# Two activation buffers declared ahead of the weight buffers, in an attention and MLP kernel

## What is computed

```python
q_bucket, k_bucket = (sum over 6 bits of (x @ proj > 0) * 2**bit for x in (q, k))
scores = where(q_bucket == k_bucket, q @ k.T / 8, -1e9)     # batch 2, 8 heads, 768 x 768, head_dim 64
attn = exp(scores - max); attn = attn / (sum(attn) + 1e-9)
x = (attn @ v), heads side by side                          # 1536 tokens x 512
r = maximum(x @ w_in, 0)                                    # 512 -> 2048
y = (s * r * r + b) @ w_out                                 # 2048 -> 512
out = ((y @ w1) * (y @ w2)) @ w3 @ w_out2                   # 512 -> 1024 -> 1024 -> 512
```

## Time and profile before

| | us |
|---|---|
| median of 3 executions | 785.99 |
| lowest, highest | 784.29, 786.78 |
| profiled execution, its own time | 785.99 |
| its span in the profile | 784.2 |

### The profile page before, as it was taken

One profiled execution on the slowest core, in us unless ns is written; L12 is line 12 of the kernel. 1 busy time (PEld: TensorE's weight loads), 2 busy tenths in 40 slices (PEclk: granted clock), 3 DMA queues, 4 the chain that ended last, 5 costly groups with the idle time before them and its releaser, 6 DMA issues.

```text
span 784.2 us, 11231 instructions
## 1 busy us (share of the span) xinstructions
PE 756.1 (96%) x3680; PEld 625.5 (80%) x3680; DVE 459.7 (59%) x809; ACT 369.3 (47%) x686; POOL 238.9 (30%) x150
## 2 busy tenths in 40 slices
PE   3999999999989899999999999999999999999998
PEld 2788888887778778888888888888887888888886
DVE  4899999999979821277565675666675201210220
ACT  2889998898879933353232232322342211211211
POOL 3347665575566663662021020210112000000000
PEclk9999999999989999999999999999999999999999
DMA  5353334333532223233010110101010000001001
GB/s 148 80 119 82 87 91 113 78 83 85 120 114 61 67 91 107 81 109 106 1 53 1 54 54 0 53 1 53 1 53 1 1 35 20 1 14 40 0 0 54
DMA packets 17680, 45.37 MB, mean 58 GB/s; under 512 B 4946, under 2 KB 6994, under 8 KB 17650
## 3 DMA queue, kind: packets, MB, share of 16 engines
q1 hardware_dynamic: 17650, 44.99, 20.7%
HBM read 37.75 MB, written 3.19 MB: 52 GB/s over the span
## 4 chain that ended last, share of the span: by engine, by line
PE 81%; DVE 7%; ACT 4%; issue 4%; DMA 2%; SPq 1%; POOL 0%; DVEq 0%; ACTq 0%
PE psum L986 54%; PE psum L1073 8%; PE psum L940 6%; PE psum L927 5%; PE psum L916 3%; DVE top L745 3%; PE psum L910 3%; ACT prob L524 2%; DVE pt_lo L759 1%; ACT pt_hi L540 1%; DVE x_lo L863 1%; PE psum L901 1%; DMA stage<-in_w_out 1%; DMA raw<-in_qk 1%; DVE qm L738 1%
## 5 line engine op out<-in xcount | busy, mean ns | idle before, releaser
L759 DVE TENSOR_TENSOR pt_lo<-psum,pt_hi 128x384 fp32r<-128x384 f32 x192 | 97.8, 549 | 12.7 <-ACT pt_hi L540 11.2
L524 ACT ACTIVATE prob<-psum,exp_at 128x768 f32<-128x768 f32 x96 | 96.3, 1003 | 11.2 <-DVE exp_at L752 11.1
L540 ACT ACTIVATE pt_hi<-psum 128x384 fp32r<-128x384 f32 x192 | 84.3, 494 | 20.3 <-PE psum L927 18.9
L745 DVE TENSOR_REDUCE top<-psum 128x1 f32<-128x768 f32 x96 | 90.9, 947 | 4.2 <-PE psum L916 4.0
L632 ACT ACTIVATE relu<-psum 128x512 f32<-128x512 f32 x48 | 28.6, 598 | 131.4 <-PE psum L986 131.4
L986 PE MATMUL psum<-x_hi,w_c 128*128 128x512 f32 (+1 forms) x288 | 88.7, 389 | 0.0
L986 PE MATMUL psum<-x_hi,w_b 128*128 128x512 f32 (+1 forms) x288 | 88.7, 389 | 0.0
L927 PE MATMUL psum<-ident,prob 128*128 128x128 f32 x576 | 83.8, 280 | 4.2 <-DVE pt_lo L759 3.9
L886 DVE TENSOR_TENSOR ab<-psum,a_sb 128x512 f32<-128x512 f32 x24 | 16.6, 691 | 117.8 <-ACT a_sb L682 117.8
L840 DVE SCALAR_TENSOR_TENSOR relu<-psum,relu 128x512 f32<-128x512 f32 x48 | 33.1, 689 | 84.8 <-ACT relu L632 79.8
L403 POOL TENSOR_TENSOR w_b<-stage,w_b 128x1024 fp32r<-128x1024 f32 x18 | 43.7, 2427 | 122.9 <-ACT w_b L551 122.2
(11 more groups left out here) (91 smaller groups left out, 1460.0 us busy)
## 6 DMA issues: line engine op xcount, KB each, us to landing
raw<-in_qk SPq DMA_DIRECT2D x30, 384.0 KB, 5.2
stage<-in_w_out SPq DMA_DIRECT2D x12, 512.0 KB, 3.3
stage<-in_w3t SPq DMA_DIRECT2D x8, 512.0 KB, 3.9
stage<-in_w_in SPq DMA_DIRECT2D x8, 512.0 KB, 3.2
stage<-in_w SPq DMA_DIRECT2D x8, 512.0 KB, 3.3
raw_v<-in_v SPq DMA_DIRECT2D x16, 192.0 KB, 2.7
qm<-both_hi SPq DMA_DIRECT2D x16, 192.0 KB, 2.7
r_sb<-r_rows SPq DMA_DIRECT2D x16, 192.0 KB, 5.4
```

The source lines that it names most:

```text
L524: act.activation(prob[:, t % 3], score[t % 2], ACT.Exp, bias=exp_at[:, t % 2, 1:2], scale=exp_at[:, t % 2, 0:1], accum_out=rsum[:, (t // 6 ...
L540: act.activation(pt_hi[:, u % 2, 3 * part:3 * part + 3, (t % 3) * P:(t % 3 + 1) * P], turned[part].rearrange("p (j q) -> p j q", j=3), ACT ...
L745: dve.tensor_reduce(top[:, t % 2, 1:2], score[t % 2], AX.X, ALU.max, negate=True).then_inc(top_done, 1)
L759: dve.tensor_tensor(pt_lo[at], turned[part].rearrange("p (j q) -> p j q", j=3), pt_hi[at].bitcast(F32), ALU.subtract).then_inc(pt_lo_done, 1)
```

## The change

Two declarations move from behind w_b to the head of the list. x_hi then begins at byte 16,512, x_lo at 41,088, stage at 65,664, ident at 73,856, sb_col at 74,368, w_a at 74,400 and w_b at 107,168. Before, stage began at 16,512, ident at 24,704, sb_col at 25,216, w_a at 25,248, w_b at 58,016, x_hi at 74,400 and x_lo at 98,976. The next buffer begins at 123,552 in both.

```diff
+        x_hi = sb("x_hi", [P, KT, TOK], FR)
+        x_lo = sb("x_lo", [P, KT, TOK], FR)
         stage = sb("stage", [P, 2, WCH], F32)
         ident = sb("ident", [P, P], F32)
         sb_col = sb("sb_col", [P, 2], F32)
         w_a = sb("w_a", [P, 8 * WCH], FR)
         w_b = sb("w_b", [P, 4 * WCH], FR)
-        x_hi = sb("x_hi", [P, KT, TOK], FR)
-        x_lo = sb("x_lo", [P, KT, TOK], FR)
```

## The result

| | before | after |
|---|---|---|
| median of 6 executions, us | 785.13 | 792.94 |
| lowest to highest, us | 783.85 to 786.78 | 791.89 to 794.51 |
| profiled execution, us | 785.99 | 792.57 |
| its span, us | 784.2 | 790.8 |

The kernel is slower by 0.98%: ratio 1.0098, 95% interval 1.0083 to 1.0113, 7.8 us. The forecast was no change.

What follows compares the result with a forecast made beforehand. PE was taken to bound the kernel from 279.5 us on, at 226.7 ns per matmul. All six terms were 0, so 785.99 + 0 = 786.0 us, range 782.6 to 789.0, no change at 0.82.

Steps and rivals of the forecast that it cites:

- What bounds the kernel: PE sets the end from 279.52 us on; 2208 matmuls at 226.7 ns make 500.6 of 504.7 us, hand-over the rest.
- The alignment step: Buffer starts: only x_hi and x_lo change alignment, from 32 past a multiple of 64 onto one; five others keep theirs.
- Term 1: 1152 matmuls streaming x_hi or x_lo, hidden steps and second part: 0, between 15.4 us gained and 16.1 us lost.
- Terms 2 to 6: Weight loads, x_hi/x_lo writes at the hand-over, ACT copies, transfers into stage, register arithmetic for x addresses: each 0.
- The rule weighed: Skill's 215.7 ns per 512-column matmul against 226.7: if start address cost it, 12.7 us gain; 16-byte lines said no change.
- rival A: 64-byte start makes streamed x reads cheaper: in whole 770.6 us, chance 0.03; in part 780.9 us, chance 0.03.
- Rival B: Hidden steps: x directly below busy stage makes 576 matmuls 14 ns longer each, 8.1 us lost, 794.1 us; chance 0.05.
- The sign I had named: MLP matmuls: forecast wrong if paces streaming x and g differ by 2 ns or more; 1152 x 2 ns is 2.3 us.

Runs made afterwards that it cites:

- Experiments 1, 2 and 4: 1: 32-byte pads around x_hi/x_lo, either layout, 792.92 and 793.89 us; 2: one front pad 786.77, shifted x views 791.54; 4: changed kernel, sb_col ahead of x_hi, 784.82.
- experiment 7: Also spelled stream_alone: separate kernel with only matmuls on constant data; total time meaningless; float32r, 512 columns: 226.7 ns at distance 0, 233.4 at 32 and 128.
- low_32: Changed kernel with 32-byte pads ahead of x_hi and behind x_lo, so x begins 32 bytes further up: 792.92 us, ratio 1.0097 to the kernel before.

## Why the prediction was wrong

- **What bounds the kernel** held. PE sets the end from 278 us on, and 1152 of the 2208 matmuls carry the change. One reading in it was loose: the hand-over is 11.3 us of the chain (584.27 to 595.61), not the 4.1 that 504.7 - 500.6 leaves, as 48 of the x matmuls run beside it.
- **The alignment step** failed first. I worked out that 57,888 bytes leave a remainder of 32 modulo 64 and that the weights move by a multiple of 256, and took the streamed operand's own alignment for what could matter. The two moved by different remainders modulo 256 (-32 and 0), and that relation is what costs. Experiments 1, 2 and 4 show it: all operands on a multiple of 64 is fast, the same x address is fast or slow by its weights. (Stage is also not the only one of the five that a transfer fills, sb_col is another; nothing hung on that.)
- **Term 1** is the step that failed in the sum. Its value of 0 came from rows with four streamed buffers and three weight buffers, all at 389 ns. They looked like many placements and were one: every one began at 160 modulo 512. What was constant in them was the very thing that the change altered. The term was 6.7 ns x 1152 = 7.7 us; the upper bound of 16.1 us, borrowed from ACT copies, held it, but I let the range end at 789.0.
- **Terms 2 to 6** held. Weight loads read 188 ns, the hand-over, the ACT copies and the hole at 218 us were the same, and the register-addressed blocks lose 6.7 ns per matmul beside 6.3 (0.91 us over 144) in the one with fixed addresses.
- **The rule weighed.** The Trainium skill's 215.7 ns (TensorE: Matmul & The Clock Gate, section "Wait — 56ns, not 53.3ns?") agrees with this chip for bfloat16: 215.8 ns in experiment 7. For float32r no distance tried gave a pace under 226.7, so those 11 ns were not to be had by moving buffers; rival A was as wrong as the forecast. The 16-byte lines that the Trainium skill states (SBUF — State Buffer, section "Door 1: The DMA port swizzle") did not decide either: starts at 32 and at 0 modulo 256 are both on a line, and cost 233.4 and 226.7 ns.
- **Rival B** named 794.1 us and lay near the result by luck, as its mechanism was another. It had neighbours using stage while x streams, hidden steps longer and the second part unchanged. The second part lost 1.28 us a block with POOL at rest, and stream_alone lost the same with all else idle.
- **The sign I had named** for being wrong, 2 ns or more between the pace of x and of g, came: 233.3 against about 227.
- The sizes agree: 7.7 us by count against 7.8 measured. In the profiled execution some 0.5 us of the piece of 1344 falls on the 576 g matmuls, whose mean step is 227.6: only the first five after a run of x matmuls are long (228 to 236 ns), the rest take 226.7 as before. The 48 x matmuls beside the hand-over give 0.3 back.

## What to carry to other kernels

Where PE streams float32r in matmuls of 512 columns at its limit, lay out the streamed operand and its weights so that their starts agree modulo 256 bytes; 32 bytes of a small constant between two buffers cost 1% here. Before a set of equal rows is taken as proof that placement doesn't matter, work out every operand's address and see whether the rows differ in anything. A change that moves only addresses can be taken back in part by pads. But a pad moves everything declared behind it: in low_32 it gave x its old start back and took that of the weights away. So every operand's address is worked out anew for each trial.

## What was not expected of the hardware

- In an unbroken run of float32r matmuls of 128 rows and 512 columns, each with weights of its own, the pace is 226.7 ns when streamed operand and weights start equal modulo 256 bytes, and 229 to 236 ns otherwise, most of them 233 to 234 (stream_alone and the kernels agree); there is no effect in bfloat16 (215.8 to 216.0 ns at five distances).
- The effect depends on the width: +6.7 ns at 512 columns and distance 128, +1.1 at 448, +2.2 at 384, and -2.5 at 256, where distance 0 is the slower one, in one execution of stream_alone.
- The Trainium skill (SBUF — State Buffer, section "Who interferes with whom") gives PE two read ports for SBUF, one for the streamed operand and one for weights, and calls them independent. In these runs the pace depends on how the two operands lie to each other. The measurement decides that they are not without effect on each other in float32r; where in the engine they meet is open, as is why a matmul is long both for its own weights and for the next. A float32r weight load takes 188 to 190 ns of the 226.7, a bfloat16 one 98 of the 215.8, where the distance costs nothing. Whether it is the length of the load that counts no run shows, since the streamed type changed with it.
